# Attention in 64-token blocks on quarters of the TensorE array, with outputs turned by transposes

## The chip, the cores and the metric

The kernel runs on one core of a Trainium2 chip. The metric is the device time of one execution in microseconds (us), lower is better. The core's engines are TensorE (PE in the profile, its weight loads PEld), VectorE (DVE), ScalarE (ACT), GpSimd (POOL) and the DMA queues, most of them issued by SyncE (SP). All run their own instruction streams and meet at semaphores.

## What is computed

Decayed linear attention over 2 batches, 8 heads, 768 tokens of 64 features, then a token-mixing and channel MLP block, then a Fourier mixing block with an MLP. The change touches the attention alone:

```python
for b in range(nb):                      # blocks of 64 tokens
    intra = einsum('bhic,bhjc->bhij', qb, kb) * Dmask   # lam ** (i - j) where i >= j
    intra = einsum('bhij,bhjd->bhid', intra, vb)
    inter = einsum('bhid,bhde->bhie', qb * lam_pow, kv_state)     # lam ** (i + 1)
    out[:, :, sl] = intra + inter
    kv_state = lam ** block * kv_state + einsum('bhsd,bhse->bhde', kb * rev_pow, vb)
x = out as (batch, 768, 512)
u = x + (relu(x.T @ w_tok1) @ w_tok2).T
x = u + relu(u @ w_ch1) @ w_ch2
u = x + real(fft(fft(x, axis=1), axis=2));  un = layernorm(u)
return u + relu(un @ w2_ch1) @ w2_ch2
```

The block size is free: the same sums come out with blocks of 128 tokens, if mask and powers go by 128.

## The kernel before

All of it is written by hand, engine by engine, with counting semaphores; no scheduler moves anything. The tokens of the second half lie in the order 0, 127, 126, ... 1 inside each chunk of 128, in q and in the outputs, which the Fourier stage wants. That is why operations on them are split into chunks 0 to 2 (`NA`) and 3 to 5.

Attention runs head by head in chunks of 128 tokens (`NC` = 6), both batches side by side. In round h TensorE issues, in this order:

- `scores(h + 1)`: 12 matmuls, keys by queries, 64 rows by 128 columns of the array each; batch 0 on the upper 64 rows, batch 1 on the lower (line 1177);
- `state_products(h + 1)`: 10 matmuls, `kdec` by `vns`, 128 rows by 64 columns, one batch in each column half (line 1165);
- the products of `qdec` with `state`, 10 matmuls of 64 rows by 128 columns (line 1210);
- the products of the masked scores `pt` with `vns`, 12 matmuls on the whole array (line 1216). They end in `att_done`.

Each of these fp32 matmuls shows as two weight loads and two matmuls in the trace. Outputs have tokens on partitions, as the token mixing wants them.

VectorE does `mask(h)` (scores times mask, out of PSUM), `states(h)` (a copy and four chained steps) and `decay_q(h)`, and builds three of the decay masks by doubling (line 739). GpSimd builds the other five (lines 335 and 340). ScalarE builds the rows of powers by doubling, seven steps a head (`decay_row`), scales k (`decay_k`) and copies each head's outputs twice, as `xh` and `u` (line 470 is the helper of all ScalarE copies). The semaphore `u_placed` tells that a head is placed. Inputs come through SP into rings of three heads; a ring place is loaded again when its reader has reported.

After the last head the token mixing begins (line 1237), with `xh` as moving operand. It starts the dense part of the kernel, in which nothing is changed.

## Time and profile before

| | |
|---|---|
| median of 3 runs | 592.2 us (589.27 to 592.4) |
| profiled execution | 589.51 us, its span 587.7 us |
| busy share of the span | PE 97%, PEld 87%, DVE 63%, ACT 45%, POOL 45% |
| attention | from the first loads to 59.91 us, where the token mixing's first weights are loaded |
| one round of attention | 6.35 us |

The span is the profiler's time from the first to the last instruction; 1.8 us lie around it. PE time is shown as busy while a matmul is in its pipeline, so overlapping matmuls make a busy share near 100%; how far starts lie apart says more.

### The profile page before, as it was taken

The page shows a single profiled execution, that of the slowest core. Times are in us where ns is not written, and L with a number is a line of the kernel's source. Part 1 is how long each engine was busy: PE and PEld are TensorE (multiplying, and loading weights), DVE is VectorE, ACT ScalarE, POOL GpSimd, SP SyncE. Part 2 cuts the span into 40 slices and gives each one's busy share as a digit, 9 for nine tenths or more (in the row PEclk, how much of TensorE's full clock was granted, in tenths as well). Part 3 has the DMA queues.
Part 4 walks back from the last instruction along what each step waited for, and adds up shares of the span by engine and source line. Part 5 has one row for each costly group of instructions (what it writes and reads, how often), then busy time and mean ns, then how long its engine had stood idle before and what let it go on. Part 6 is the DMA issues. An engine that isn't in the chain of part 4 may idle for free.

```text
span 587.7 us, 9130 instructions
## 1 busy us (share of the span) xinstructions
PE 572.7 (97%) x3330; PEld 509.1 (87%) x3330; DVE 371.8 (63%) x676; ACT 263.7 (45%) x558; POOL 266.1 (45%) x298
## 2 busy tenths in 40 slices
PE   8999999999999998999989989999999999999997
PEld 6999887888899987899868878998798989899996
DVE  7987847776654695366978953678765644443323
ACT  6676315556544443343454433434544443444330
POOL 6884235366553463314656632237655233333311
PEclk9999999999999999999999989999999999999999
DMA  8880110322222211120212111202122222111232
GB/s 308 303 339 28 72 37 1 126 99 88 76 74 70 72 60 32 55 72 22 69 55 71 35 56 55 71 20 69 58 72 71 72 72 72 63 59 48 67 143 108
DMA packets 24158, 49.10 MB, mean 84 GB/s; under 512 B 2473, under 2 KB 3633, under 8 KB 24113
## 3 DMA queue, kind: packets, MB, share of 16 engines
q1 hardware_dynamic: 23520, 46.70, 23.3%
q0 software_dynamic: 448, 1.71, 1.0%
q8 instruction: 27, 0.44, 0.3%
q14 instruction: 19, 0.15, 0.1%
q10 hardware_dynamic: 144, 0.10, 0.1%
HBM read 45.35 MB, written 3.15 MB: 83 GB/s over the span
## 4 chain that ended last, share of the span: by engine, by line
PE 79%; DVE 13%; POOL 3%; issue 2%; ACT 2%; DMA 0%; DVEq 0%; ACTq 0%; POOLq 0%
PE banks L1154 13%; PE banks L1155 13%; PE banks L1153 13%; PE banks L1385 10%; PE banks L1387 10%; PE banks L1388 10%; PE banks L1216 3%; PE banks L1210 2%; PE banks L1226 1%; DVE u L936 1%; DVE al L731 1%; PE banks L1177 1%; DVE e L731 1%; POOL tl L355 1%; POOL raw L355 1%
## 5 line engine op out<-in xcount | busy, mean ns | idle before, releaser
L355 POOL TENSOR_TENSOR w2l<-raw,w2h 128x512 fp32r<-128x512 f32 x56 | 75.0, 1340 | 165.0 <-ACT w2h L470 165.0
L1385 PE MATMUL banks<-th,al 128*128 128x384 f32 x392 | 132.7, 338 | 4.9 <-DVE snap L1053 2.2
L1387 PE MATMUL banks<-tl,ah 128*128 128x384 f32 x392 | 132.2, 337 | 0.0
L1388 PE MATMUL banks<-th,ah 128*128 128x384 f32 x392 | 132.0, 337 | 0.0
L470 ACT ACTIVATE snap<-banks 128x384 f32<-128x384 f32 x84 | 41.2, 490 | 133.4 <-PE banks L1388 127.3
L731 DVE TENSOR_TENSOR al<-raw,ah 128x512 fp32r<-128x512 f32 (+1 forms) x112 | 89.6, 821 | 4.8 <-ACT ah L470 3.9
L1053 DVE TENSOR_TENSOR snap<-banks,snap 128x384 f32<-128x384 f32 x84 | 46.4, 552 | 65.2 <-PE banks L1388 64.8
L1385 PEld LDWEIGHTS banks<-th,al 128*128 128x128 f32 x392 | 73.6, 188 | 15.4 <-issue 4.0
L1387 PEld LDWEIGHTS banks<-tl,ah 128*128 128x128 f32 x392 | 73.6, 188 | 5.8
L1388 PEld LDWEIGHTS banks<-th,ah 128*128 128x128 f32 x392 | 73.6, 188 | 0.0
L355 POOL TENSOR_TENSOR raw<-raw 128x256 f32<-128x256 f32 x84 | 69.3, 841 | 2.2
L839 DVE SCALAR_TENSOR_TENSOR h0l<-snap,h0h 128x384 fp32r<-128x384 f32 x56 | 36.4, 650 | 50.8 <-ACT h0h L660 50.6
L1153 PE MATMUL banks<-w2h,h1l 128*128 128x512 f32 x168 | 67.1, 399 | 0.2 <-POOL w2l L355 0.2
L1155 PE MATMUL banks<-w2h,h0h 128*128 128x512 f32 x168 | 66.5, 396 | 0.0
L1154 PE MATMUL banks<-w2l,h0h 128*128 128x512 f32 x168 | 66.3, 395 | 0.0
L1155 PE MATMUL banks<-w2h,h1h 128*128 128x512 f32 x168 | 66.2, 394 | 0.0
L1154 PE MATMUL banks<-w2l,h1h 128*128 128x512 f32 x168 | 66.0, 393 | 0.0
L1153 PE MATMUL banks<-w2h,h0l 128*128 128x512 f32 x168 | 65.8, 391 | 0.2 <-DVE u L872 0.2
L470 ACT ACTIVATE ah<-raw 128x512 fp32r<-128x512 f32 (+1 forms) x112 | 61.0, 568 | 2.8 <-POOL raw L355 2.8
L368 POOL TENSOR_TENSOR raw<-raw 128x256 f32<-128x256 f32 x28 | 22.1, 790 | 74.5 <-DVE al L731 39.1
L355 POOL TENSOR_TENSOR tl<-sums,th 128x512 fp32r<-128x512 f32 (+1 forms) x21 | 35.8, 1729 | 27.8 <-ACT th L470 27.8
L660 ACT ACTIVATE h0h<-snap 128x384 fp32r<-128x384 f32 x56 | 29.2, 521 | 20.7 <-DVE snap L1053 20.7
(179 smaller groups left out, 943.0 us busy)
## 6 DMA issues: line engine op xcount, KB each, us to landing
raw<-w1b_dram SPq DMA_DIRECT2D x16, 512.0 KB, 3.2
raw<-w2b_dram SPq DMA_DIRECT2D x32, 256.0 KB, 2.8
raw<-w1a_dram SPq DMA_DIRECT2D x12, 512.0 KB, 3.2
raw<-w2a_dram SPq DMA_DIRECT2D x24, 256.0 KB, 3.2
kTs<-kT_dram SPq DMA_DIRECT2D x8, 384.0 KB, 5.9
qTs<-qT_dram SPq DMA_DIRECT2D x8, 384.0 KB, 6.8
kns<-kn_dram SPq DMA_DIRECT2D x8, 384.0 KB, 7.2
vns<-vn_dram SPq DMA_DIRECT2D x8, 384.0 KB, 5.0
```

The lines of the kernel that those rows point to most:

```text
L355: return nc.gpsimd.tensor_tensor(o, i0, i1, ALU.subtract)
L470: return nc.scalar.activation(o, i, ACTF.Copy, **kw)
L660: nc.scalar.activation(o, src, ACTF.Relu).then_inc(hh_ready, 1)
L731: return nc.vector.tensor_tensor(o, i0, i1, ALU.subtract)
L839: return nc.vector.scalar_tensor_tensor(out=o, in0=src, scalar=0.0, in1=f(hi), op0=ALU.max, op1=ALU.subtract)
L1053: nc.vector.tensor_tensor(snap[:, i, :], bank[7][:, 0:HALF], snap[:, i, :], ALU.add).then_inc(x_ready, 1)
L1153: mm(o, ll, rh_, start=start, stop=False)
L1154: mm(o, lh, rl_, start=False, stop=False)
L1155: return mm(o, lh, rh_, start=False, stop=stop)
L1385: mm(o[:, 0:HALF], al[:, a, cols], th[b][:, t, k, :], start=start and k == 0, stop=False, skip_group_check=True)
L1387: mm(o[:, 0:HALF], ah[:, a, cols], tl[b][:, t, k, :], start=False, stop=False, skip_group_check=True)
L1388: last = mm(o[:, 0:HALF], ah[:, a, cols], th[b][:, t, k, :], start=False, stop=(k == 1), skip_group_check=True)
```

## The change

Blocks are of 64 tokens now: each chunk of 128 is two halves e = 0, 1. Every attention matmul is 64 by 64 with 64 moving columns, on one quarter of the array.

- Scores: 24 matmuls a head, in the order chunk, batch, half. The four of a chunk lie on four different quarters.
- State products: 22 a head, again four quarters in turn; states of all 12 blocks are kept.
- Output products: operands are swapped, so that features are on partitions. 24 products with the masked scores (line 1181) come first, in four quarters; then 22 of `qdec` with `state` (line 1193), batch 0 on the first quarter and batch 1 on the last only.
- `output_columns(h)` on ScalarE copies the result out of PSUM (384 + 384 + 3 elements a partition), `turn(h)` transposes it with six 128 by 128 transposes on TensorE, and ScalarE copies those (768 elements) to `xh` and to `u`.
- `decay_q` moves to GpSimd; a small GpSimd copy puts the first token of a chunk behind its last (`first_token`), so q needs a row length of 129 and its loads fall into runs of 128 elements.
- Masks and rows of powers are 64 wide, made by one scan each on VectorE. The doubling steps on three engines are gone.
- `states(h)`: ScalarE scales the first halves' products; VectorE adds, does four chained 64-wide steps and one 384-wide step.
- Products of k and v, scores and outputs have one PSUM buffer each, where the k-v products had two.

The parts that the numbers hang on; `decay_q` is GpSimd's now, `output_columns` and the loop with `decay_k` ScalarE's, `decay_rows` and the state steps VectorE's, the last loop TensorE's.

```diff
+            def decay_q(h):
+                pool.wait_ge(row_ready, h + 1)
+                pool.wait_ge(q_ready0, h + 1)
+                if h >= 2:
+                    pool.wait_ge(att_done, h - 1)
...
+                for chunks, first, r in ((slice(0, NA), 0, row), (slice(NA, NC), 1, row[:, ::-1])):
+                    last = nc.gpsimd.tensor_tensor(
...
+            def output_columns(h):
+                act.wait_ge(att_done, h + 1)
+                if h >= 2:
+                    act.wait_ge(otr_done, h - 1)
+                o = oT[:, h % 2, :, :]
+                there = o[:, :, 1:L + 1].rearrange("p c (s i) -> p c s i", s=2)
+                copy(there[:, :, 0:NA, :], outs[:, :, 0:NA, :])
+                copy(there[:, :, NA:NC, :], outs[:, ::-1, NA:NC, :])
+                copy(o[:, NA:NC, 0:1], outs[:, 0, NA:NC, D - 1:D]).then_inc(ot_ready, 1)
...
             for h in range(H):
-                if h + 2 < H:
-                    decay_row(h + 2)
-                    decay_k(h + 2)
+                output_columns(h)
+                if h + 2 < H:
+                    scale_first_half(h + 2)
+                cols = slice(h * D, (h + 1) * D)
+                act.wait_ge(otr_done, h + 1)
+                copy(xh[:, :, cols].rearrange("p (b s) d -> p s b d", b=B), turned)
+                copy(u[:, :, cols].rearrange("p (b s) d -> p s b d", b=B), turned).then_inc(u_placed, 1)
+                if h + 3 < H:
+                    decay_k(h + 3)
+                elif h == H - 3:
                     act.wait_ge(s_tokw, 32)
                     copy(t1h[:, :, :], t1raw[:, :, :]).then_inc(tok1h, 1)
...
+            def decay_rows(h):
+                base = lamb[:, h:h + 1].to_broadcast([L, D])
+                nc.vector.tensor_tensor_scan(dmask[:, h, :], base, eyes[:, :], 0.0, ALU.mult, ALU.add).then_inc(dmask_ready, 1)
+                nc.vector.tensor_tensor_scan(lrow[:, h, :], base, ident[:, 0:D], 1.0, ALU.mult, ALU.add).then_inc(row_ready, 1)
...
+                link(nc.vector.tensor_tensor(st[:, 0, 1:NC, :], st[:, 0, 1:NC, :], kv[1][:, 0:NC - 1, :], ALU.add))
+                for c in range(2, NC):
+                    link(nc.vector.scalar_tensor_tensor(out=st[:, 0, c, :], in0=st[:, 0, c - 1, :], scalar=lam128[:, h:h + 1],
+                                                        in1=st[:, 0, c, :], op0=ALU.mult, op1=ALU.add))
+                nc.vector.scalar_tensor_tensor(out=st[:, 1, :, :], in0=st[:, 0, :, :], scalar=lam64, in1=kv[0],
+                                               op0=ALU.mult, op1=ALU.add).then_inc(state_ready, 1)
...
             for h in range(H):
                 if h + 1 < H:
                     scores(h + 1)
-                    if h:
-                        state_products(h + 1)
+                    state_products(h + 1)
+                pe.wait_ge(mask_done, 2 * (h + 1))
+                if h:
+                    pe.wait_ge(ot_ready, h)
+                for c in range(NC):
+                    for e in range(2):
+                        for b in range(B):
+                            there, rows = slice(D * e, D * (e + 1)), slice(D * b, D * (b + 1))
+                            last = mm(bank[4 + e][rows, c * D:(c + 1) * D], vns[there, h % NI, c, rows],
+                                      pt[there, h % 2, b, c, :], start=(c == 0), stop=False, skip_group_check=True)
+                last.then_inc(intra_done, 1)
+                if h:
+                    turn(h - 1)
...
+            turn(H - 1)
```

On TensorE, a round in the middle of the attention stands so before (tensors are written `out<-moving,weights`; `attention_in_residual` is `u_placed`):

```order
L1177 MATMUL banks<-qTs,kTs 128x128 [waits mask_done,qT_kT_loaded_1]
L1177 MATMUL banks<-qTs,kTs 128x128 x5
L1177 MATMUL banks<-qTs,kTs 128x128 [waits mask_done]
L1177 MATMUL banks<-qTs,kTs 128x128 x5
L1165 MATMUL banks<-vns,kdec 64x64 [waits state_ready,v_loaded_1,kdec_ready]
L1165 MATMUL banks<-vns,kdec 64x64 x9
L1210 MATMUL banks<-state,qdec 128x64 [waits attention_in_residual,qdec_ready,state_ready]
L1210 MATMUL banks<-state,qdec 128x64 x9
L1216 MATMUL banks<-vns,pt 128x64 [waits mask_done]
L1216 MATMUL banks<-vns,pt 128x64 x2
```

And the same round of the changed kernel:

```order
L1142 MATMUL banks<-qTs,kTs 64x64 [waits mask_done,first_token_of_q_placed,qT_kT_loaded_1]
L1142 MATMUL banks<-qTs,kTs 64x64 x23
L1128 MATMUL banks<-vns,kdec 64x64 [waits state_ready,v_loaded_1,kdec_ready]
L1128 MATMUL banks<-vns,kdec 64x64 x21
L1181 MATMUL banks<-pt,vns 64x64 [waits output_columns_copied,mask_done]
L1181 MATMUL banks<-pt,vns 64x64 x23
L1153 MATMUL banks<-ident,oT 128x128 [waits attention_in_residual,output_columns_copied]
L1153 MATMUL banks<-ident,oT 128x128 x5
L1193 MATMUL banks<-qdec,state 64x64 [waits intra_block_done,qdec_ready,state_ready]
L1193 MATMUL banks<-qdec,state 64x64 x21
```

44 matmuls a head have become 92 and six transposes, the products with the masked scores now stand ahead of those with the state, and they wait for ScalarE's copy of the previous head.

On ScalarE, one head before (the seven steps of `decay_row`, then k, then the outputs):

```order
L470 ACTIVATE lrow<-lrow,lp 128x16 [waits lam_row_step]
L470 ACTIVATE lrow<-lrow,lp 128x32 [waits lam_row_step]
L470 ACTIVATE lrow<-lrow,lp 128x64 [waits lam_row_step]
L470 ACTIVATE kdec<-kns,lrev 128x768 [waits kv_done,k_loaded_2]
L470 ACTIVATE xh<-banks 128x6x64 [waits attention_done]
L470 ACTIVATE u<-banks 128x6x64
```

And one head after:

```order
L468 ACTIVATE oT<-banks 128x2x3x64 [waits output_transposed,attention_done]
L468 ACTIVATE oT<-banks 128x2x3x64
L468 ACTIVATE oT<-banks 128x3
L468 ACTIVATE state<-banks,lrow 128x5x64 [waits attention_done,lam_row_ready,kv_done]
L468 ACTIVATE xh<-banks 128x6x2x64 [waits output_transposed]
L468 ACTIVATE u<-banks 128x6x2x64
L468 ACTIVATE kdec<-kns,lrev 128x768 [waits kv_done,k_loaded_0]
```

The output passes ScalarE twice: once as columns, before the transposes, and once after them, and the k of a later head stands between one head's second pass and the next head's first.

## Rows read from the trace of the kernel before

**Rows 1.** Windows: busy time of each engine (x instructions), granted clock, DMA share, GB/s

```profile
36.91:43.27 6.36, 6.36 (x89) 6.03 (x89) 4.56 (x12) 5.15 (x14) 5.50 (x12) 1.00 0.84 306
55.98:59.91 3.93, 3.93 (x45) 3.86 (x44) 2.80 (x2) 3.12 (x5) 0.00 (x0) 1.00 0.00 0
```

**Rows 2.** Timeline of weight loads over one round: start, length, engine, line, operation

```profile
24.21 1.42 PEld L1177 LDWEIGHTS banks<-qTs,kTs 64*128 64x128 f32 x24
25.75 0.66 PEld L1165 LDWEIGHTS banks<-vns,kdec 128*64 128x64 f32 x20
26.48 1.19 PEld L1210 LDWEIGHTS banks<-state,qdec 64*128 64x128 f32 x20
27.74 2.75 PEld L1216 LDWEIGHTS banks<-vns,pt 128*128 128x128 f32 x24
```

**Rows 3.** Windows of 30 ns, line 1165 alone: PE busy (x), PEld busy (x)

```profile
25.74:25.77 0.03, 0.02 (x2) 0.02 (x2) 1.00 0.25 102
25.77:25.80 0.03, 0.03 (x2) 0.03 (x2) 1.00 0.50 205
25.80:25.83 0.03, 0.03 (x2) 0.03 (x4) 1.00 0.76 205
```

**Rows 4.** Groups by form, 0 to 60 us: busy, mean ns of one

```profile
L1165 PEld LDWEIGHTS banks<-vns,kdec 128*64 128x64 f32 x160 | 5.3, 137 | 1.2 <-ACT kdec L470 0.4
```

**Rows 5.** Timeline: transposes of the MLP stage, and the ScalarE copies behind them

```profile
86.56 1.90 PEld L1226 LDWEIGHTS banks<-ident,u 128*128 128x128 f32 x16
...
87.43 0.81 ACT L470 ACTIVATE sums<-banks 128x768 f32<-128x768 f32 x1 [10.26 <-PE banks L1226]
88.14 2.21 ACT L470 ACTIVATE th<-banks 128x768 fp32r<-128x768 f32 x3
```

**Rows 6.** Timeline of ScalarE and of TensorE's first load of the token mixing

```profile
35.85 0.94 ACT L470 ACTIVATE kdec<-kns,lrev 128x768 f32<-128x768 f32 x1 [2.06 <-DMA kns<-kn_dram]
...
36.69 0.47 ACT L470 ACTIVATE xh<-banks 128x384 fp32r<-128x384 f32 x1
...
37.06 0.48 ACT L470 ACTIVATE u<-banks 128x384 f32<-128x384 f32 x1
...
50.49 1.49 ACT L470 ACTIVATE t1h<-raw 128x1536 fp32r<-128x1536 f32 x1
...
59.91 0.19 PEld L1237 LDWEIGHTS banks<-xh,t1l 128*128 128x128 f32 x1
```

**Rows 7.** Groups by form on VectorE

```profile
L1053 DVE TENSOR_TENSOR snap<-banks,snap 128x384 f32<-128x384 f32 x84 | 46.4, 552 | 65.2 <-PE banks L1388 64.8 <-ACT snap L470 0.3
L807 DVE SCALAR_TENSOR_TENSOR state<-state,lp,banks 128x64 f32<-128x64 f32 x32 | 9.0, 281 | 1.1
L772 DVE TENSOR_TENSOR qdec<-qTs,lrow 128x3 f32<-128x3 f32 x8 | 3.0, 370 | 0.0
```

**Rows 8.** Groups by form on GpSimd

```profile
L355 POOL TENSOR_TENSOR w2l<-raw,w2h 128x512 fp32r<-128x512 f32 x56 | 75.0, 1340 | 165.0 <-ACT w2h L470 165.0
L355 POOL TENSOR_TENSOR raw<-raw 128x256 f32<-128x256 f32 x84 | 69.3, 841 | 2.2
```

**Rows 9.** Timeline of the start

```profile
4.10 1.66 POOL L321 TENSOR_TENSOR lp<-lamb,ex 128x8 f32<-128x8 f32 x1 [3.65 <-DMA ex<-expo_dram]
...
15.29 0.94 ACT L470 ACTIVATE kdec<-kns,lrev 128x768 f32<-128x768 f32 x1 [0.60 <-DMA kns<-kn_dram]
...
17.14 1.42 PEld L1177 LDWEIGHTS banks<-qTs,kTs 64*128 64x128 f32 x24
```

**Rows 10.** Windows, columns as in rows 1

```profile
10.00:20.00 10.00, 9.48 (x140) 8.80 (x139) 9.47 (x27) 8.14 (x22) 8.61 (x18) 1.00 1.03 411
...
338.90:342.40 3.50, 1.71 (x8) 1.01 (x6) 3.40 (x6) 1.59 (x4) 2.48 (x3) 1.00 0.13 49
342.70:346.10 3.40, 3.40 (x12) 3.30 (x12) 1.41 (x2) 1.97 (x5) 2.03 (x3) 0.51 0.33 77
346.10:349.50 3.40, 3.40 (x19) 3.19 (x18) 1.50 (x3) 0.57 (x2) 0.00 (x0) 1.00 0.00 0
```

More of the change, by code:

```diff
@@ L98, in build @@
         ring, att = ExitStack(), ExitStack()
-        qTs = sb(ring, "qTs", [L, NI, S])
+        qTs = sb(ring, "qTs", [L, NI, NC, L + 1])
         kTs = sb(ring, "kTs", [L, NI, S])
@@ L351, in _ @@
+            for h in range(H):
+                decay_q(h)
+                if h + 2 < H:
+                    first_token(h + 2)
             pool.wait_ge(tok1h, 1)
@@ L499, in _, with scale_first_half @@
+            def scale_first_half(h):
+                act.wait_ge(kv_done, h + 1)
+                act.wait_ge(row_ready, h + 1)
+                if h >= 2:
+                    act.wait_ge(att_done, h - 1)
+                st = state[:, h % 2, :, :].rearrange("p (c e) d -> p e c d", e=2)
+                copy(st[:, 0, 1:NC, :], bank[2][:, 0:(NC - 1) * D].rearrange("p (c d) -> p c d", c=NC - 1),
+                     scale=lrow[:, h, D - 1:D]).then_inc(kv_scaled, 1)
             act.wait_ge(lrev_ready, 1)
@@ L764, in decay_q @@
-            def decay_q(h):
-                dve.wait_ge(s_qk[h % NI], loaded(h))
-                dve.wait_ge(row_ready, h + 1)
-                if h >= 2:
-                    dve.wait_ge(att_done, 2 * (h - 1))
-                q = qTs[:, h % NI, :].rearrange("p (c i) -> p c i", c=NC)
-                for chunks, there, here in order:
-                    row = lrow[:, h, here]
-                    last = nc.vector.tensor_tensor(qdec[:, h % 2, chunks, there], q[:, chunks, there],
-                                                   row.unsqueeze(1).to_broadcast([L, NA, row.shape[-1]]), ALU.mult)
-                last.then_inc(qdec_ready, 1)
+            def decay_rows(h):
+                base = lamb[:, h:h + 1].to_broadcast([L, D])
+                nc.vector.tensor_tensor_scan(dmask[:, h, :], base, eyes[:, :], 0.0, ALU.mult, ALU.add).then_inc(dmask_ready, 1)
+                nc.vector.tensor_tensor_scan(lrow[:, h, :], base, ident[:, 0:D], 1.0, ALU.mult, ALU.add).then_inc(row_ready, 1)
@@ L782, in mask @@
             def mask(h):
-                if h in POOL_MASKS:
-                    dve.wait_ge(pmask_ready, POOL_MASKS.index(h) + 1)
+                dve.wait_ge(sc_done, h + 1)
+                dve.wait_ge(dmask_ready, h + 1)
                 if h >= 2:
-                    dve.wait_ge(att_done, 2 * (h - 1))
-                for half in range(2):
-                    dve.wait_ge(sc_done, 2 * h + half + 1)
-                    sc = banks[:, 2 * half:2 * half + 2, 0:HALF].rearrange("p b (c i) -> p b c i", c=NA)
-                    for chunks, there, here in order[:1] if half == 0 else order[1:]:
-                        d = dmask[:, h % 3, here]
-                        last = nc.vector.tensor_tensor(
-                            pt[:, h % 2, :, chunks, there], sc[:, :, :, there],
-                            d.unsqueeze(1).unsqueeze(1).to_broadcast([L, B, NA, d.shape[-1]]), ALU.mult)
-                    last.then_inc(mask_done, 1)
+                    dve.wait_ge(att_done, h - 1)
@@ L801, in states @@
                 dve.wait_ge(kv_done, h + 1)
-                for c in range(NC - 1):
-                    kv = bank[4 + h % 2][:, c * D:(c + 1) * D]
-                    if c == 0:
-                        last = nc.vector.tensor_copy(state[:, h % 2, 0, :], kv)
-                    else:
-                        last = nc.vector.scalar_tensor_tensor(
-                            out=state[:, h % 2, c, :], in0=state[:, h % 2, c - 1, :],
-                            scalar=lp[:, 7, h:h + 1], in1=kv, op0=ALU.mult, op1=ALU.add)
-                    if c < NC - 2:
-                        link(last)
@@ L1188, in _ @@
             for i in range(WARM):
-                last = mm(bank[7][:, 0:(NC - 1) * D], state[:, 0, 0:2, :], state[:, 0, :, :], start=True, stop=True)
+                last = mm(bank[7][:, 0:(NC - 1) * D], state[:, 0, 0:2, :], state[:, 0, 0:NC - 1, :], start=True, stop=True)
             last.then_inc(warm_done, 1)
@@ L1212, in _ @@
-                for b in range(B):
-                    for c in range(NC):
-                        if b == 0 and c % NA == 0:
-                            pe.wait_ge(mask_done, 2 * h + c // NA + 1)
-                        last = mm(bank[out_bank(h, b)][:, slot(c) * D:(slot(c) + 1) * D], pt[:, h % 2, b, c, :],
-                                  vns[:, h % NI, c, D * b:D * (b + 1)], start=False, stop=True, skip_group_check=True)
-                    last.then_inc(att_done, 1)
-                if h == 0:
-                    state_products(1)
+                pe.wait_ge(intra_done, h + 1)
@@ new lines, in _ @@
+                for c in range(NC):
+                    for e in range(0 if c else 1, 2):
+                        for b in range(B):
+                            rows = slice(D * b, D * (b + 1))
+                            last = mm(bank[4 + e][rows, c * D:(c + 1) * D], state[rows, h % 2, 2 * c + e, :],
+                                      qdec[rows, h % 2, c, half_of(c, e), :], start=False, stop=True, skip_group_check=True)
+                last.then_inc(att_done, 1)
+            turn(H - 1)
```

236 lines of the change are left out of this document (95 added, 141 removed).

## The prediction

> **What bounds the kernel now.** I read windows first, one for each round of attention. In a round TensorE is busy 6.36 of 6.36 us while VectorE has 4.56, ScalarE 5.15 and GpSimd 5.50 us of work, and the clock is full [rows 1]. Six rounds follow each other at 6.35 us, and the token mixing's first weights go in at 59.91 [rows 6], directly behind the last round of 3.93 us [rows 1]. So attention is bound by TensorE, and from 59.91 on the program is the same in both kernels. The whole question is at what time the changed kernel comes to that load.
>
> The timeline of weight loads says what TensorE spends a round on: 24 loads of the scores from 24.21, 20 of the state products from 25.75, 20 of 64 by 128 from 26.48, 24 of the whole array in 2.75 us from 27.74 [rows 2]. On the whole array a load takes 115 ns (2.75 / 24). The 64 by 128 ones come in pairs, about 112 ns a pair (from 24.21 to the next stage at 25.75 are 1.54 us; less 0.2 for the change of array shape, / 12). The 128 by 64 ones take 58 ns a pair: (0.66 - 0.137) / 9 with the length of one, 137 ns [rows 2, 4]. A 30 ns window at the head of the stage has two loads and two matmuls, the next has no further one, and the one after that has four loads [rows 3]. So the two parts of the array do load and multiply together; time goes with columns loaded in one part (about 0.9 ns each, two passes) and is shared between parts that are free.
>
> **The change, TensorE.** Four quarters in turn have 64 columns each. If all four run together, four records (a load and its matmul) take 58 ns, 14.5 each. Then scores cost 48 x 0.0145 = 0.70 us, state products 44 x 0.0145 = 0.64, products with the masked scores 0.70. The products with the state use two quarters only, so 29 ns a record: 44 x 0.029 = 1.28. Six transposes at 119 ns (1.90 / 16 [rows 5]) are 0.71. Changing the shape costs what the next stage is late by: 26.48 - 25.75 = 0.73, less 10 pairs of 0.058, is 0.15, and I take 0.2 [rows 2]; there are two changes a round where there were four, 0.4. Sum 4.43 us against 6.35. The bounds of a record: 14.5 ns, and 29 ns if quarters pair up only as halves did; then the three stages cost 0.69 + 0.64 + 0.69 more and the sum is 6.45. I take 14.5, since the halves' time followed the columns and not the number of instructions: the 64 by 128 pair took 112 and the 128 by 64 pair 58 with the same number of records.
>
> A rule of the Trainium skill speaks against that (TensorE: Matmul & The Clock Gate, Part 1): matmuls do not start closer than about 25 ns however small they are. By it the sum would be 140 x 0.025 + 1.28 + 0.71 + 0.4 = 5.89. Rows 3 have two starting within one 30 ns window and none in the next, which neither shows nor excludes a floor on the mean.
>
> **The change, the ring over ScalarE.** TensorE at 4.43 is not the round. The products with the masked scores wait for `ot_ready` of the previous head, ScalarE gives that only after the copies of the head before that and after `decay_k`, and those copies wait for the transposes, which stand behind the products. Once around: copy to `xh` 0.71 and to `u` 0.71 (88.14 - 87.43, 768 elements from PSUM [rows 5]); `kdec` 0.84 (36.69 - 35.85 [rows 6]); two copies of 384 at 0.37 (37.06 - 36.69) and a tiny one, between 0.1 and 0.37, together 0.95; handover 0.05; products 0.70; change of shape 0.2; six transposes and their end 1.0 (four took from 86.56 to 87.43, 0.87, of which some 0.2 went by behind a wide matmul, plus two more [rows 5]). Sum 5.16 us. That is my round: 1.2 us less than now, with TensorE idle 0.7 of it. With 29 ns a record the ring is 5.85, below TensorE's 6.45.
>
> **Others in a round.** VectorE: mask 2 x 0.55 (line 1053 is the nearest form [rows 7]), add 0.5 and last step 0.6 (estimates from the same form), four chained steps 4 x 0.31 (0.28 [rows 7] and the handover), two scans. No row has a scan; 64 wide it costs no less than the 64-wide step's 0.28 [rows 7] and I allow twice that, taking 0.28. Sum 4.0, at most 4.6. GpSimd: `decay_q` is two products of 384 elements, between 0.84 (256 wide) and 1.34 (512) [rows 8], I take 1.1: 2.4 with the small copy, ahead of its use by most of a round. Masks and powers by doubling (up to seven steps a head on ScalarE, fourteen on GpSimd) go, but their cover was TensorE's 6.36, so they give nothing themselves. `states(h)` ends 1.0 us before the next state products need their single buffer. Loads: a head's 1.57 MB take 3.8 us at 411 GB/s [rows 10], below 5.16. q now falls into runs of 512 bytes; that costs from nothing to another 0.96 us a head (its 0.39 MB once more), still hidden in the rounds and open at the start only.
>
> **The start.** k of head 2 reaches ScalarE at 15.29 when the DMA engines are saturated (share 1.03) [rows 9, 10]; three loads of q in short runs put it 0 to 2.9 us later, I take 1. `lrev` comes first now, at 4.1 + 0.2 + 1.66 [rows 9], and VectorE is freed of the doubling, but `decay_q(0)` stands behind the 1.66 of a power and behind q of head 1. States of head 0 are ready near 12.9, the state products of head 1 wait for them (single buffer), and output products end near 16.1: 12.9 + 0.64 + 0.70 + 0.3 + 1.28 + 0.3. Round 1 began at 17.14 before [rows 9], so 1 us is won there. k of head 2 (16.3 + 0.84) delays the first output copy, so the first transposes reach ScalarE at about 20.0.
>
> **The end.** From 20.0, five rounds of 5.16 give 45.8. In the next, `t1h` with 1.49 stands where `kdec` had 0.84 [rows 6]: +5.8, 51.6. Now the chain lies open: two copies 1.42, output columns of the last head 0.95, handover 0.05, transposes 1.0, two copies 0.71 + 0.81: 56.5. Before, the last head was copied batch by batch under TensorE's work. So this tail eats about 3.5 us of the 7 us that seven shorter rounds and the start win. 59.91 - 56.5 = 3.4 us earlier.
>
> **The clock.** In that tail TensorE idles about 1.2 us, works 0.8, idles 1.6. The only place in the old trace with so little work is 338.9 to 342.4: busy 1.71 of 3.5 us, after which the clock was at half (1.2 GHz, granted 0.51) for 3.4 us, in which 12 matmuls began where 19 did in the next 3.4 us [rows 10]. 7 x 0.18 = 1.3 us lost. I expect this at the head of the token mixing. Net gain 2.1 us, and 589.5 becomes 587.4. The profiled run is 2.7 us below the median of the three runs; on the median's scale the same gain is 592.2 - 2.1 = 590.1. I predict 590.
>
> **Rivals**, each as a change to 589.5.
>
> - The clock stays up: -3.4. For it: a single place in the rows shows a fall, so I can't say how much idling it takes; against: the tail idles more than that place did [rows 10].
> - Quarters pair up only as halves do (29 ns a record). Output products of head 0 end near 17.3, six rounds of 6.45 give 56.0, and behind it the open chain, 10.2 (less the 1.28 already gone by for the transposes, then 5.77 + 0.69 + 4.99): 66.2, +6.3, with the clock +7.6, 597. The order on the engine puts both passes of one fp32 matmul on the same quarter next to each other, which could hold up the next quarter; rows 3 speak against it, since pairs there begin together. This is the case on the other side; it decides once a record costs over 20 ns, where TensorE's sum passes the ring's.
> - A fixed spacing of starts between the two, 25 ns: sum 5.9 a round, attention ends at 62.4, +2.5, with the clock +3.8. The skill's page named above states such a floor.
> - VectorE's chained steps and GpSimd's `decay_q` hold each other up. Three elements took VectorE 370 ns on average in `decay_q`, line 772 [rows 7], beside GpSimd's work. The new chained steps and scans read two SBUF operands. If both 1.1 us products of GpSimd fall on them, VectorE's round is 4.0 + 2.2 = 6.2, over 5.16: five rounds cost 5 more, +3. I place `decay_q` at 0 to 2.3 us after `att_done` of its ring place and the chain at 2.5 to 4.8, so they just miss; it decides from 1.1 us of slip.
>
> **How the numbers follow.** Chances: forecast 0.50, clock stays 0.15, pairs only 0.12, fixed spacing 0.10, hold-up 0.08, others such as q's loads or late instructions 0.05. About 0.5%, 3 us, is what a measurement of this kernel can tell from no change. Faster by more: most of the clock case (0.12) and the lower part of the forecast's spread, which is +-1.5 us for 0.3 us a round unknown (0.12): 0.24. Slower by more: pairs 0.12, spacing 0.08, hold-up 0.04, others 0.02: 0.26. The rest, 0.50, within. The forecast's own range is 587.5 to 592; to hold 8 in 10 it must go up into the spacing and pair cases and down to the profile's scale with the clock up: 585.8 to 597.
>
> **What would show it.** Scores: 48 loads in about 0.8 us (0.7 and the last one's length), or 1.4 in the pairs case. Weight loads of the scores from round to round 5.2 apart. ScalarE with hardly any idle time between `u` and the next output columns, and TensorE waiting on ScalarE's `oT` for 0.7 us a round. First token-mixing load near 56.5. VectorE's 64-wide chained steps at about 0.3 each; if they are near 0.8, the hold-up is real. A granted clock of about 0.5 for 3.4 us near 57 to 60. Wrong would be above all: a record over 20 ns, or ScalarE's copies with features split by batch costing more than the plain rows.

## The result, and the profile after

The changed kernel takes 606.5 us (median of four runs, 605.3 to 609.0), the kernel before 591.3 (four runs, 589.3 to 592.4): a ratio of 1.027, with an interval of 1.022 to 1.031. It is 15 us slower, where I predicted 590 and a range up to 597. Its profiled execution has a span of 603.4 us.

Nearly all of it arises in the attention. The first load of the token mixing, line 1213 now, stands at 74.44 us; it was at 59.91 [rows 6], and I had it at 56.5. That is 14.5 of the 15.7 us between the two profiled spans; the other 1.2 come behind it, where the granted clock is 0.50 for a while (shown below).

Timeline of TensorE's weight loads in the changed kernel, from the end of one round to the next but one. In brackets is the idle time ahead of a row and what ended it; `issue` means that no semaphore in the profile explains it.

```profile
23.10 0.80 PEld L1181 LDWEIGHTS banks<-pt,vns 64*64 64x64 f32 x48
23.96 0.64 PEld L1153 LDWEIGHTS banks<-ident,oT 128*128 128x128 f32 x6
24.77 1.06 PEld L1193 LDWEIGHTS banks<-qdec,state 64*64 64x64 f32 x33 [0.17 <-issue]
27.73 0.36 PEld L1193 LDWEIGHTS banks<-qdec,state 64*64 64x64 f32 x9 [1.90 <-issue]
...
29.42 0.44 PEld L1181 LDWEIGHTS banks<-pt,vns 64*64 64x64 f32 x24
31.38 0.44 PEld L1181 LDWEIGHTS banks<-pt,vns 64*64 64x64 f32 x24 [1.52 <-issue]
...
38.08 0.67 PEld L1128 LDWEIGHTS banks<-vns,kdec 64*64 64x64 f32 x40 [2.70 <-issue]
...
44.46 0.42 PEld L1193 LDWEIGHTS banks<-qdec,state 64*64 64x64 f32 x11 [3.12 <-issue]
...
48.12 0.48 PEld L1181 LDWEIGHTS banks<-pt,vns 64*64 64x64 f32 x25 [1.49 <-issue]
```

Each stage is as fast as predicted: 48 loads in 0.80 us, where 24 took 2.75 [rows 2]. But the engine stops *inside* stages, between matmuls that wait for nothing: after 33 of the 44 loads of the products with the state, after 24 of the 48 of the products with the masked scores. Count the loads between two stops. From 27.73 to the stop ahead of 31.38 there are the last 11 with the state (9 in the row, two among the rows left out), 48 of the scores, 44 state products and 24 with the masked scores, 127; then 24 + 6 + 44 + 48 + 4 = 126 to the one ahead of 38.08. Each load has its matmul, so the stops are some 253 instructions apart, wherever in the code that falls. Here is what the list of waits puts down to it on the weight-load side, 15 to 75 us:

```profile
PEld banks L1181 <- issue: 7.5, 5, 2.6
PEld banks L1193 <- issue: 7.0, 11, 3.1
PEld banks L1128 <- issue: 5.1, 3, 2.7
```

That is 19.6 us. Of this, 2.6 us are one wait for ScalarE's `oT`, which ends at 66.12 (on the matmul side of the same instructions the list names it), and about 1.6 us are changes of array shape, 0.17 or 0.33 each. Some 15 us of stops are left. Windows over two rounds of the changed kernel, columns as in rows 1:

```profile
33.92:44.75 10.83, 4.99 (x197) 4.34 (x195) 4.73 (x10) 4.91 (x9) 2.17 (x4) 1.00 0.89 315
44.75:50.70 5.95, 4.60 (x197) 4.22 (x196) 3.65 (x10) 2.58 (x6) 1.88 (x2) 1.00 0.77 255
```

The first round is 10.83 us long, though no engine has as much as 5 us of work in it (before: 6.36, all of it TensorE's [rows 1]). Where TensorE was busy throughout, no engine is now.

### The profile page after: what moved, and what is told of

It reads as the page before. It is cut to its first block, busy times and chain, and to the rows that moved or that the text cites. A ratio compares the mean times of both kernels' runs of the same rounds, so it can differ in the third digit from the quotient of the medians.

```text
span 603.4 us, 10660 instructions
## 1 busy us (share of the span) xinstructions
PE 565.2 (94%) x4146; PEld 498.2 (83%) x4146; DVE 357.8 (59%) x643; ACT 256.3 (42%) x517; POOL 246.6 (41%) x250
## 2 busy tenths in 40 slices
DMA packets 29281, 49.18 MB, mean 82 GB/s; under 512 B 2472, under 2 KB 9776, under 8 KB 29232
## 4 chain that ended last, share of the span: by engine, by line
PE 76%; DVE 11%; issue 4%; ACT 4%; POOL 3%; DVEq 0%; ACTq 0%; POOLq 0%
PE banks L1116 12%; PE banks L1117 12%; PE banks L1115 12%; PE banks L1361 10%; PE banks L1363 9%; PE banks L1364 9%; PE banks L1202 1%; PE banks L1193 1%; DVE u L898 1%; DVE al L733 1%; PE banks L1128 1%; PE banks L1181 1%; PE banks L1153 1%; DVE e L733 1%; POOL tl L353 1%
```

## The experiments

My theory, "blocks" below: TensorE's instructions arrive in blocks of 256, a block takes over 3.5 us to get, and quarter matmuls use it up in half of that. The trace of the changed kernel suggests it in one more view, the transfers: 33 instruction packets of the kind q8 in the whole program, 0.54 MB or 16 KB each, where the kernel before has 27. TensorE's matmuls and loads are 8292 in the one and 6660 in the other; divided by 256 and rounded up, that is 33 and 27. The same division gives the number of q8 packets of every other trace shown below, but for experiment 7, whose trace has 26 where 27 are due. So q8 carries TensorE's instructions, 256 to a packet. The rivals: "places" (the stops belong to certain matmuls, by a conflict of quarters, a drain, the clock) and "loads" (q's 512-byte pieces, which raise the packets under 2 KB from 3633 to 9776, starve the engines).

### 1. The same program, shifted by 64 instructions

```diff
             keep_warm(1)
+            for _ in range(16):
+                mm(bank[7][:, 0:1], ident[:, 64:64 + L], ident[:, 64:65], start=True, stop=True)
             state_products(0)
```

> The changed kernel with 16 more matmuls of one column on TensorE in the idle time before the first products (64 instructions: 32 loads and 32 matmuls). Theory 'blocks' (TensorE's instructions arrive in blocks of 256, and the pauses are waits for the next block): the pauses stay at the same counts of weight loads from the start of the program (about 222, 348, 475, 602, 728), now counted with the added 32, so each comes 32 loads earlier in the program's work; time the same within 2 us. Rival 'places' (the pauses belong to certain matmuls: quarters in conflict, a drain between accumulation groups, the clock): the pauses stay at the same matmuls, so the counts become 254, 380, 507, 634, 760.

Measured, 611.3 us in one run. Timeline of weight loads (line 1195 is line 1193 of the changed kernel):

```profile
25.67 0.64 PEld L1153 LDWEIGHTS banks<-ident,oT 128*128 128x128 f32 x6
26.47 0.13 PEld L1195 LDWEIGHTS banks<-qdec,state 64*64 64x64 f32 x1 [0.17 <-issue]
30.07 2.10 PEld L1195 LDWEIGHTS banks<-qdec,state 64*64 64x64 f32 x38 [3.48 <-issue]
```

The stop that came after 33 loads of the products with the state now comes after one: 32 loads earlier in the program, just the number added. Three later ones keep their counts as well (475, 728, 854 and 1107 loads from the start, in both kernels). "Places" is out. The time was not the same within 2 us, as I had expected: this one run is 5 us above the changed kernel's median. The stops don't explain that. From 26 us on there are four, of 3.48, 2.98, 2.50 and 2.17 us, 11.1 together, where the changed kernel has eight with 13.6; those at 602, 981, 1233 and 1360 loads are gone. Two other things are longer. The added matmuls did not fit in the idle time: the first state products begin at 13.84, where they began at 11.76. And behind the long stops the granted clock is low, 0.50 from 30.07 to 32.40 and 0.54 from 40.43 to 43.69, where in the changed kernel it is 1.00 from 16 to 67 us. Where in a round a block ends matters by some us; why these stops are so long I can't derive.

### 2. No loads for heads 3 to 7

```diff
-            return 32 * (h // NI + 1)
+            return 32
...
+                if p >= 0:
+                    continue
                 sp.dma_start(kTs[:, i, :], kT[h]).then_inc(s_qk[i], 16)
```

The heads 3 to 7 work on the data of heads 0 to 2; GpSimd waits for the readers of its place in the ring instead.

> The changed kernel without the loads of q, k and v for heads 3 to 7, which use the data of heads 0 to 2 again (so it leaves out reading these heads). Theory 'blocks': pauses stay, one every 126 or 127 weight loads, but none of 2 to 3 us; where TensorE has work without a wait each block takes 3.66 us, so pauses of 1.2 to 1.8 us; token mixing starts at 66 to 69 instead of 74.4. Rival 'loads' (the data loads in 512-byte pieces are the cause, by starving instruction fetches or the engines): the pauses vanish and token mixing starts at 57 to 60. Rival 'places': unchanged pauses, 74.

Measured, 597.9 us in one run, token mixing from 68.38. The DMA view from 24 to 60 us, and three stops of the same stretch:

```profile
DMA packets 11, 0.16 MB, mean 5 GB/s; under 512 B 0, under 2 KB 0, under 8 KB 0
## 3 DMA queue, kind: packets, MB, share of 16 engines
q8 instruction: 9, 0.15, 1.8%
```

```profile
31.22 0.44 PEld L1179 LDWEIGHTS banks<-pt,vns 64*64 64x64 f32 x24 [1.25 <-issue]
...
39.64 0.42 PEld L1191 LDWEIGHTS banks<-qdec,state 64*64 64x64 f32 x11 [0.65 <-issue]
...
43.08 0.48 PEld L1179 LDWEIGHTS banks<-pt,vns 64*64 64x64 f32 x25 [1.26 <-issue]
```

This is the cleanest view of the mechanism. In 36 us nothing is moved but instructions: nine packets of 16 KB, and two smaller ones of another instruction queue (q14). In the same window TensorE ran 1088 matmuls and 1087 loads, 2175 instructions, or 242 to a packet (waits, and the few records that a trace lacks, are not in that number). The stops are still there, 0.5 to 1.3 us each, with a round of 5.96 us ((56.39 - 32.54) / 4 between rows of the same stage). "Loads" is out as the cause, but it is a part: without them the stops of 2.7 and 3.1 us shrink to 0.5 and 0.65, and attention is 6 us shorter. (One stop is longer, the one at 348 loads, 2.16 us where it was 1.06; I can't say why.)

### 3. Streams of matmuls without waits, after all other work

```diff
             for n in range(12):
                 down(NP - 1, n)
+            pe.wait_ge(o_added, 4 * NC + 1)
+            for n in range(160):
+                r, w = D * (n % 2), D * (n // 2 % 2)
+                mm(bank[6 + n % 2][w:w + D, 0:D], ident[r:r + D, D:2 * D], ident[r:r + D, D:2 * D], start=True, stop=True,
+                   skip_group_check=True)
...
```

> The changed kernel with four streams of matmuls without waits after all its work, no loads in flight: 160 on quarters with 64 columns, 160 on halves (128 rows, 64 outputs) with 64 columns, 96 on the whole array with 64 columns, 160 on quarters with 128 columns (4 instructions each). Theory 'blocks': the quarters of 64 columns run at 14.6 ns a record for 128 records (1.9 us) and pause for 1.8 us, so 640 instructions take 640 / 256 x 3.66 = 9.2 us; halves at 29 ns fill 3.7 us with a block and show pauses under 0.2 us, 9.3 us in all; the whole array has none; quarters of 128 columns like the halves. Rival 'places' (semaphores, accumulation groups or operands of the attention code): quarters run through in 320 x 14.6 = 4.7 us. Rival 'loads': the same 4.7 us, as nothing is loaded.

```profile
600.20 3.00 PEld L1478 LDWEIGHTS banks<-ident 64*64 64x64 f32 x198 [1.27 <-DVE u L1106]
604.47 1.94 PEld L1478 LDWEIGHTS banks<-ident 64*64 64x64 f32 x122 [1.27 <-issue]
606.48 0.31 PEld L1481 LDWEIGHTS banks<-ident 128*64 128x64 f32 x6
607.93 9.29 PEld L1481 LDWEIGHTS banks<-ident 128*64 128x64 f32 x314 [1.14 <-issue]
617.29 21.51 PEld L1483 LDWEIGHTS banks<-ident 128*128 128x128 f32 x192
638.87 8.72 PEld L1486 LDWEIGHTS banks<-ident 64*64 64x64 f32 x320
```

Quarters of 64 columns (line 1478) run at 15 ns a record (3.00 / 198) and stop after 198 and after another 122 + 6 = 128 records, which are 256 instructions; from one resumption to the next are 3.46 us. Halves (line 1481) take 29.6 ns a record, use up a block in 3.8 us, and don't stop in 314. Nor do quarters with 128 columns (line 1486) at 27 ns, 3.5 us a block, over 320 records; but that is only two and a half blocks, behind a slow stream. So it isn't the quarters as such: it is how fast instructions are used. The first stream took 6.2 us (600.20 to 606.41) and not the 9.2 that I expected: it ran 198 records before its first stop and had one stop inside. That instructions had been gathered in the idle time ahead of it is my reading; no row shows it.

### 4. The same streams beside loads

Three streams of 256 quarter products; the first alone, the second beside 24 loads of whole rows of 3 KB, the third beside 24 loads of the same rows in pieces of 512 bytes.

```diff
+                    if k:
+                        sp.dma_start(o.rearrange("p (c n) -> p c n", c=NC)[:, :, 0:L],
+                                     qT[n % H].rearrange("p (c n) -> p c n", c=NC)).then_inc(s_load[k][i], 16)
+                    else:
+                        sp.dma_start(o, qT[n % H]).then_inc(s_load[k][i], 16)
```

> The changed kernel with three streams of 256 quarter products (1024 instructions, four blocks, no waits) after all its work: the first with no loads in flight, the second beside loads of whole rows of 3 KB (24 of 384 KB, three in flight), the third beside the same loads in pieces of 512 bytes. Theory 'blocks, held up by loads': 3.5 us from one resumption to the next in the first, 4 to 5 us in the second, 5 to 6 us in the third. Rival (the longer pauses in attention had another reason than the loads): 3.5 us in all three.

```profile
608.16 1.96 PEld L1498 LDWEIGHTS banks<-ident 64*64 64x64 f32 x128 [1.18 <-issue]
611.89 1.96 PEld L1498 LDWEIGHTS banks<-ident 64*64 64x64 f32 x128 [1.77 <-issue]
615.62 1.00 PEld L1498 LDWEIGHTS banks<-ident 64*64 64x64 f32 x58 [1.77 <-issue]
...
625.44 1.96 PEld L1498 LDWEIGHTS banks<-ident 64*64 64x64 f32 x128 [0.94 <-issue]
629.44 1.96 PEld L1498 LDWEIGHTS banks<-ident 64*64 64x64 f32 x128 [2.04 <-issue]
...
658.19 1.96 PEld L1498 LDWEIGHTS banks<-ident 64*64 64x64 f32 x128 [0.35 <-issue]
663.29 2.93 PEld L1498 LDWEIGHTS banks<-ident 64*64 64x64 f32 x128 [3.14 <-issue]
```

A block of 256 instructions runs in 1.96 us and is followed by a stop. Start to start: 3.73 us with nothing else going on (615.62 - 611.89, and the one before), 4.00 beside whole rows, 5.10 beside pieces of 512 bytes. That last is one interval; the next is 4.55, with the clock in part at half, so below the 5 to 6 us that I expected. The Trainium skill (Runtime: NRT & Kernel Launch, "Instruction fetch mechanics") says that an engine's instructions are refilled in blocks of 256, 16 KiB each, by a queue of the sequencer's own while the current block runs; that agrees with 128 records a stretch and 16 KB a packet. It also calls the cost of a block's end mostly hidden, and gives TensorE an instruction memory of 2048 instructions; neither shows in these streams, where TensorE, after the first 198 records, stops at every block.

### 5. One pass in place of two

```diff
-                            last = mm(bank[2 + e][rows, c * D:(c + 1) * D], kdec[there, h % 2, c, rows],
-                                      vns[there, h % NI, c, rows], start=True, stop=True, skip_group_check=True)
+                            last = mm(bank[2 + e][rows, c * D:(c + 1) * D], hi(kdec[there, h % 2, c, rows]),
+                                      hi(vns[there, h % NI, c, rows]), start=True, stop=True, skip_group_check=True)
```

The same for the scores and both products of the outputs; `hi` is a view of the upper 16 bits.

> The changed kernel with attention's products on the upper halves of its operands (bfloat16 views): one load and one matmul each in place of two and two, so a round has some 200 instructions instead of 380 (precision is left out; every wait, product and copy stays). Theory 'blocks': one block a round or less, hidden like in the kernel before; rounds of 5.2 us by the ring over ScalarE, token mixing from 56 to 60. Rival 'places': pauses of 1 to 3 us stay at the same products, token mixing at 68 or later.

Measured, 596.3 us in one run, token mixing from 63.2. Of the stops inside stages two are left, of 1.82 and 0.80 us. A round, from one head's scores at 24.77 to the next at 30.11, is 5.34 us:

```profile
24.77:30.11 5.34, 3.57 (x110) 2.93 (x104) 2.88 (x8) 3.57 (x8) 2.02 (x3) 0.50 0.80 259
```

TensorE waits in it for `kdec` and `oT` of ScalarE and ScalarE for the transposes, so it is the ring; but the clock is at half (granted 0.50), and that nearly holds from 19 to 67 us (0.56 from 19 to 45, 0.51 from 45 to 63.2). So this run changed two things, the number of instructions and, without my asking for it, the clock, and it can't be set beside the changed kernel without that. From the first transpose to ScalarE's copy go 1.58 us here and 0.92 in the changed kernel.

And 63.2 is later than the 56 to 60 that I expected. Against the 56.5 of the prediction, 4.4 us are the start: ScalarE's first copy behind transposes begins at 24.37, predicted 20.0. Five rounds from there take 27.3 us (predicted 25.8) and the rest 11.5 (10.7), with the clock low in both. What follows 63.2 also takes 2.2 us longer than in the changed kernel. A further part of the lateness can be read off VectorE and GpSimd:

```profile
44.46 3.68 POOL L333 TENSOR_TENSOR qdec<-qTs,lrow 128x384 f32<-128x384 f32 x4
...
45.63 2.91 DVE L779 SCALAR_TENSOR_TENSOR state<-state,lam 128x64 f32<-128x64 f32 x4
...
49.33 0.53 PE L1131 MATMUL banks<-vns,kdec 64*64 64x64 bf16 x22 [2.82 <-DVE state L781]
...
51.09 1.25 DVE L779 SCALAR_TENSOR_TENSOR state<-state,lam 128x64 f32<-128x64 f32 x4
```

Four chained steps of VectorE take 2.91 us beside `decay_q` and 1.25 without it; TensorE waits 2.82 us for them. This is my hold-up rival. Five of the eight heads have it in this run (1.77 to 2.91 us), and TensorE waits for it twice, 5.3 us in all; in the changed kernel one head has it (2.33 us at 40.15).

### 6. q in whole rows

```diff
-                sp.dma_start(qTs[:, i, :, 0:L], qT[h].rearrange("p (c n) -> p c n", c=NC)).then_inc(s_qk[i], 16)
+                sp.dma_start(qTs[:, i, 0:S], qT[h]).then_inc(s_qk[i], 16)
```

> The changed kernel with q loaded in whole rows of 3 KB in place of 768 pieces of 512 bytes a head; the last query column of chunks 3 and 4 then holds the next chunk's first token, which is the part of the computation that is changed. Theory 'blocks': the pauses stay at the same counts of loads; those of 2.7 to 3.1 us shrink by the congestion that the small pieces caused; token mixing starts 1 to 4 us earlier than 74.4; ratio to the kernel before 1.020 to 1.026. Theory 'small pieces are the cause': token mixing at 60 to 64, ratio under 1.008.

Measured: ratio 1.0235 (1.020 to 1.027), token mixing from 72.51, nearly all stops at the counts where they were. So the small pieces cost 1.9 us by the traces, half of it at the start: k of head 0 reaches ScalarE at 7.35 instead of 9.48, and ScalarE's first copy behind the transposes begins at 23.82 instead of 24.88. Of the two longest stops one shrank, as I had expected, from 3.12 to 1.01 us, and the other did not (2.70 before, 2.97 now). So data loads lengthen stops in large pieces as well.

### 7. Scans alone, in the kernel before

```diff
-            def decay_mask(h, k0, k1):
...
+            def decay_rows(h):
+                base = lamb[:, h:h + 1].to_broadcast([L, L])
+                nc.vector.tensor_tensor_scan(dmask[:, h, :], base, ident[:, 64:64 + L], 0.0, ALU.mult, ALU.add).then_inc(dmask_ready, 1)
+                nc.vector.tensor_tensor_scan(lrow[:, h, :], base, zeros[:, :], 1.0, ALU.mult, ALU.add).then_inc(row_ready, 1)
```

> The kernel before with the decay masks and rows by scans and nothing else of the change: products in blocks of 128 tokens, TensorE's instructions as they were. Both theories: TensorE is busy in every round of the kernel before (6.35 us), and the masks and rows were made beside it, so rounds stay at 6.35 us; only the start can move, by 1 us at most. Ratio to the kernel before 1.000 (0.997 to 1.003). If the scans, or VectorE working beside GpSimd, had a part in the loss, this one would be slower too, by 0.5% or more.

Measured: ratio 0.9985 (0.9969 to 1.0001). As expected: rounds stay at 6.35 us, token mixing starts at 60.04. Neither the loss nor a gain is in the scans.

### 8. The change without its quarters

Scans, outputs with features on partitions, GpSimd's `decay_q`, all as in the change, but blocks of 128 tokens and products 128 columns long. The last head keeps the old orientation, so that no copies and transposes stand open at the end.

```diff
+                for c in range(NC):
+                    for b in range(B):
+                        rows, at = slice(D * b, D * (b + 1)), c % NA * L
+                        last = mm(bank[4 + c // NA][rows, at:at + L], vns[:, h % NI, c, rows], pt[:, h % 2, b, c, :],
+                                  start=(c % NA == 0), stop=False, skip_group_check=True)
...
+                for c in range(1, NC):
+                    for b in range(B):
+                        rows, at = slice(D * b, D * (b + 1)), c % NA * L
+                        last = mm(bank[4 + c // NA][rows, at:at + L], state[rows, h % 2, c - 1, :], qdec[rows, h % 2, c, :],
+                                  start=False, stop=True, skip_group_check=True)
```

> The change without its quarters: scans, outputs with features on partitions and transposes per chunk as in the changed kernel, but in blocks of 128 tokens, with products that are 128 columns long (98 weight loads a round in place of 190), the last head in the old orientation, so that nothing is turned at the end. Theory 'blocks' (the loss is the delivery of 380 instructions a round; the orientation itself is sound): 196 instructions a round need 2.8 us, so no pauses; a round is TensorE's sum, scores 1.42 + state products 0.66 + products of the mask 1.4 + transposes 0.64 + products of the state 1.2 = 5.3 us, with gaps 5.5; six rounds at 0.85 less than 6.35 make 5 us: ratio 0.991 (0.986 to 0.996). Rival (the turned outputs, their copies on ScalarE and GpSimd's decayed q are the loss): rounds of 6.5 us or more, ratio over 1.005.

Measured: 585.6 us, ratio 0.9923 (0.9892 to 0.9953). It beats both kernels, the one before by a little under 1%. A round of it:

```profile
40.83 1.42 PEld L1118 LDWEIGHTS banks<-qTs,kTs 64*128 64x128 f32 x24 [0.17 <-issue]
42.37 0.66 PEld L1105 LDWEIGHTS banks<-vns,kdec 128*64 128x64 f32 x20
42.94 1.30 PEld L1173 LDWEIGHTS banks<-pt,vns 128*64 128x64 f32 x24
44.41 0.64 PEld L1130 LDWEIGHTS banks<-ident,oT 128*128 128x128 f32 x6 [0.17 <-issue]
45.22 1.07 PEld L1183 LDWEIGHTS banks<-qdec,state 64*64 64x64 f32 x20 [0.17 <-issue]
...
56.82 0.19 PEld L1202 LDWEIGHTS banks<-xh,t1l 128*128 128x128 f32 x1
```

5.62 us a round (I had 5.5) with TensorE busy throughout, and no stop but for the changes of shape; in all of attention there is one longer wait, 1.03 us for a mask at 37.30. The gain over 6.35 is in the products with the masked scores: with features on partitions each needs half of the array, and two run together, 1.30 us where it took 2.75 [rows 2]; the transposes give 0.8 of it back. The granted clock is 1.00 throughout.

### 9. The same version with four times the score instructions

```diff
-                        last = mm(at_score(b, c), kTs[rows, h % NI, cols], qTs[rows, h % NI, cols], start=True, stop=True,
-                                  skip_group_check=True)
+                            for e in range(2):
+                                rows, there, at = slice(D * b, D * (b + 1)), slice(D * e, D * (e + 1)), c * L + D * half
+                                last = mm(at_score(b, c)[there, D * half:D * (half + 1)], kTs[rows, h % NI, c * L + D * e:c * L + D * (e + 1)],
+                                          qTs[rows, h % NI, at:at + D], start=True, stop=True, skip_group_check=True)
```

> The version in blocks of 128 tokens with turned outputs (ratio 0.992), with one thing changed: each score product of 128 rows and 128 columns is made as four quarter products of 64 by 64 (96 weight loads a round in place of 24; at 14.6 ns instead of 60 ns each the same 1.4 us of TensorE); data, waits, orientation and all other engines' work are the same. A round then has 170 loads in place of 98, some 345 instructions. Theory 'blocks': 232 of them are due in the 2.1 us of scores and state products, a block takes 3.5 us or more, so pauses without a releaser of up to 1.4 us, nine blocks in attention: token mixing 3 to 8 us later than its 56.8, ratio to the kernel before 0.997 to 1.006. Rival (what cost the changed kernel its time is something other than the number of instructions): no pauses, token mixing at 57, ratio 0.992.

Measured: ratio 1.0079 (1.005 to 1.011), token mixing from 65.22: 8.4 us later than in the version it was made from. One edit turns a kernel that is faster than the old one into one that is slower, by more and smaller instructions for the same products.

```profile
16.85 1.04 PEld L1120 LDWEIGHTS banks<-qTs,kTs 64*64 64x64 f32 x52
19.88 0.77 PEld L1120 LDWEIGHTS banks<-qTs,kTs 64*64 64x64 f32 x43 [1.99 <-issue]
20.73 0.66 PEld L1105 LDWEIGHTS banks<-vns,kdec 128*64 128x64 f32 x20
21.30 2.32 PEld L1175 LDWEIGHTS banks<-pt,vns 128*64 128x64 f32 x24
...
31.61 1.63 PEld L1120 LDWEIGHTS banks<-qTs,kTs 64*64 64x64 f32 x95
33.31 0.20 PEld L1105 LDWEIGHTS banks<-vns,kdec 128*64 128x64 f32 x4
38.11 0.62 PEld L1105 LDWEIGHTS banks<-vns,kdec 128*64 128x64 f32 x16 [4.60 <-issue]
```

The time is a little above my range, and the picture is another than I drew: not nine stops of up to 1.4 us, but two long ones, of 1.99 and 4.60 us, and one of 0.20. Rounds without a stop are 5.5 us, no longer than the 5.62 of the version with long products, so the quarter products cost TensorE nothing where it does not stop. The three stops stand 349, 728 and 1233 loads from the start, where the changed kernel, another program, has stops at 348, 728 and 1233. A long stop costs more than itself: behind the one at 19.88 the granted clock is 0.54 (near 1.2 GHz) in the window 21.3 to 23.7, and the 24 loads there take 2.32 us instead of 1.30; behind the one at 38.11 they take 2.48.

## Why the prediction was wrong

**The step that failed** is the one that made the round: "TensorE at 4.43 is not the round", and so the ring over ScalarE, 5.16 us, is. Both numbers hold. TensorE is busy 4.60 us in the round from 44.75. The ring, added from the changed kernel's own rows, is 5.05 us (an estimate: `xh` to `u` 0.71, to `kdec` 0.69, to the output columns 0.82, to the products 1.05, to the transposes 0.86, to `xh` 0.92), and where instructions are half as many it shows as 5.34 us at half the clock (experiment 5). What failed is that I asked for engines and for waits, and not whether instructions come fast enough. A round has 190 loads and 190 matmuls, one block and a half; at 3.73 us a block that makes 5.5 us even undisturbed (5.96 without loads, experiment 2), and with data loads it was 5.95 to 10.8. The undisturbed limit is the smaller part: five rounds between equal stages take 30.3 us without loads and 37.4 with them, where I had 25.8. In the kernel before a round has 178 records in 6.36 us [rows 1], so 256 of them take 9.2 us, and its trace could not show a limit of 3.7. But 380 instructions in my 4.43 us are 3.0 us a block, and in the quarter stages 1.9, denser than any row that I had, and I put "late instructions" among the others, at 0.05 together with q's loads.

**Where the 17.9 us between 56.5 and 74.44 are.** ScalarE's first copy behind the transposes began at 24.88, predicted 20.0: 4.9. From there the prediction has 36.5 us to the token mixing and the trace 49.6: 13.1 more. The stops that `issue` accounts for in that stretch, 1.90, 1.52, 2.70, 3.12, 1.49, 1.30, 0.36 and 1.19, make 13.6. They all lie in the five rounds up to ScalarE's copy of the sixth head (62.30), which are 11.6 us longer than predicted, so 2 us of them cost nothing. The other 1.5 us are in the tail, and most of it is the clock's, which fell inside the attention already and not only behind it: it is 0.70 from 66.12 to 68.46 and 0.55 from 68.46 to 70.70, and the 44 loads of the last products with the state take 2.26 us where they took 1.36. The sum is read from rows; that removing the stops would give just as much back isn't shown: with half the instructions attention ended 11.2 us earlier, not 14, and that at half the clock.

**The start** was the second wrong term. I had 1 us won; the third head's scores began at 20.51, where they were at 17.14 [rows 9]. The states of head 0, predicted ready near 12.9, end at 16.52. The main part is k of head 0: `kdec` starts at 10.78, where it was 7.50. For k of head 2 I had said that q's short runs delay it by "0 to 2.9 us", and taken 1; the first k came 2.1 us late by them (experiment 6). And the load of ScalarE's table, 1.28 us, which stood at 1.18 us ahead of the row steps, now stands behind the wait for k. TensorE idles for it, and behind that the granted clock is 0.50 from 13.23 to 15.50, where the kernel before has 1.00: the first state products take 1.35 us, the next 0.81. The last part is a stop of 0.70 us ahead of 18.46; ScalarE's copy at 24.88 has another one ahead of it, 1.06 us. ScalarE's timeline at the start, the kernel before and then the changed one:

```profile
1.18 1.28 ACT L470 ACT_TABLE_LOAD   x1 [1.18 <-PEq L1557]
```

```profile
9.48 1.28 ACT L468 ACT_TABLE_LOAD   x1 [9.48 <-DMA kns<-kn_dram]
10.78 0.94 ACT L468 ACTIVATE kdec<-kns,lrev 128x768 f32<-128x768 f32 x1
```

With the row steps the change had removed the instruction that loaded the table early. I had costed it as work hidden under TensorE.

**Right**: a quarter record at 14.5 ns (48 loads in 0.80 us, 15 ns in the streams), and with it the two rivals with slower records, 25 and 29 ns, are refuted. The Trainium skill's floor of about 25 ns from start to start (TensorE: Matmul & The Clock Gate, Part 1) doesn't hold for matmuls that go to four quarters in turn. **Right** too: that the tail lies open (last products with the state from 68.46, last transposes at 71.90, token mixing at 74.44), the clock behind it (granted 0.50 from 74.44 to 77.20, 7 matmuls, then 13; 1.2 us lost, predicted 1.3), and the hold-up of VectorE and GpSimd as a mechanism.

```profile
68.40:74.44 6.04, 3.34 (x51) 2.90 (x50) 3.04 (x2) 4.07 (x8) 0.29 (x1) 0.78 0.00 0
74.44:77.20 2.76, 2.72 (x7) 2.18 (x8) 2.76 (x2) 1.27 (x1) 0.00 (x0) 0.50 0.00 0
77.20:79.96 2.76, 2.76 (x13) 2.27 (x12) 2.76 (x4) 0.00 (x0) 0.00 (x0) 0.98 0.00 0
```

**Open**: why a block takes 3.7 us when its packet takes about 1 (1.8% of 16 engines for 36 us, by nine packets, is 1.15 us each in experiment 2, and it is 1.15 too beside loads in small pieces in experiment 4); when in a block the next one is asked for (the shifted program had fewer and longer stops, and in experiment 9 most block ends cost nothing); and how data loads lengthen it. The runs show that they do, 3.73 to 4.00 to 5.10 us, not by what path. Every run here is a traced one, so whether the stops are as long without tracing isn't shown either.

## What to carry to other kernels

When a change makes the pieces of work smaller, divide the time that you forecast for an engine's instructions by their number. Here 256 instructions took 3.5 to 3.7 us to come, 14 ns each, and once 20 ns each beside loads in small pieces. Streams that use them faster paid at every block, and a program with such stages at some of them, with no semaphore to show it. The sign is an idle time put down to `issue` inside a run of equal matmuls, at equal distances counted in instructions. The gain of an array used in parts can be had with long instructions: outputs with features on partitions and 128 columns a product made attention 3 us shorter than in the kernel before, with half as many instructions as the change. Look at the granted clock of every run before its times are compared: in two of the single runs here it was low in long stretches. And when the first small operation of an engine is removed, look at what came with it, as the table load here.

## What the hardware showed that I had not expected

- TensorE's instructions come in blocks of 256: stops 128 records apart, 3.46 and 3.73 us from resumption to resumption with no data loads, 4.00 beside loads of 3 KB rows, 5.10 and 4.55 beside loads of 512-byte pieces. Records of 29.6 ns did not outrun it over 314 records, nor records of 27 ns over 320; records of 15 ns do. The number of q8 packets is that of TensorE's instructions divided by 256 and rounded up, in ten of eleven traces.
- Beside data loads a single stop was up to 4.60 us long, and the granted clock was 0.54 behind a stop of 1.99 us and 0.50 behind one of 3.48.
- ScalarE's table load, 1.28 us, came behind the wait of the first activation: at 1.18 us where that was a small early one, at 9.48 where it was `kdec`.
- Four quarters of the array in turn take a load and a matmul every 15 ns, over 128 and in two traces 198 records in a row.
